# Moving VectorE's weight sums and accumulations, and two slices' splitting, inside the steps of a Strassen-like expert stage

## The reference, cut to what matters

```python
attn = top-32 attention of q, k, v               # 2 x 8 heads, 576 tokens, 64 columns
x    = ((attn @ w_a) * (attn @ w_b)) @ w_out     # 1152 tokens, 512 -> 1536 -> 512
p    = domain_probs / (domain_probs.sum(-1, keepdims=True) + 1e-9)
out  = 0
for e in range(4):                               # four experts, 512 -> 1024 -> 512
    h    = maximum(x @ w1[e], 0)
    out += p[:, e:e+1] * (h @ w2[e])
```

## Time and profile before

| | us |
|---|---|
| median of 3 runs (853.74 to 858.55) | 856.28 |
| the profiled execution, its own time | 848.76 |
| its span, first to last instruction | 847.0 |
| TensorE matmul busy in the span | 786.0 (93%) |
| VectorE busy | 578.2 (68%) |
| ScalarE busy | 432.8 (51%) |
| GpSimd busy | 362.5 (43%) |
| mean granted TensorE clock, share of full speed | 0.972 |

### The profile page before, as it was taken

How to read it: one execution, slowest core, us unless ns; L and a number is a source line. 1 busy time by engine, 2 the same in 40 slices (tenths; PEclk the granted TensorE clock), 3 DMA queues, 4 the chain that set the end, 5 groups by cost and what they waited for, 6 DMA issues and landing times. The chain is left out here.

```text
span 847.0 us, 14223 instructions
## 1 busy us (share of the span) xinstructions
PE 786.0 (93%) x5141; PEld 690.2 (81%) x5141; DVE 578.2 (68%) x1144; ACT 432.8 (51%) x848; POOL 362.5 (43%) x325
## 2 busy tenths in 40 slices
PE   4479899999999999999998799989999899989998
PEld 3357778888888888888897699789898799969987
DVE  6999998999999999995626544552456434472423
ACT  6677777777777777777545323332133323333211
POOL 2768764444444444445237102641044422363000
PEclk9668999999999999999999999999999999999999
DMA  9440684474545754445683003200032002210101
GB/s 242 123 145 27 219 286 151 145 209 163 172 152 174 232 193 158 159 156 195 226 272 105 1 26 83 68 26 1 25 100 75 1 1 75 79 47 1 51 1 62
DMA packets 80710, 97.94 MB, mean 116 GB/s; under 512 B 32896, under 2 KB 60032, under 8 KB 80640
## 3 DMA queue, kind: packets, MB, share of 16 engines
q1 hardware_dynamic: 79584, 96.77, 36.2%
q10 hardware_dynamic: 1056, 0.26, 0.1%
HBM read 86.00 MB, written 11.01 MB: 115 GB/s over the span
## 5 line engine op out<-in xcount | busy, mean ns | idle before, releaser
L730 PE MATMUL ps<-x_hi,w_hi 128*128 128x256 f32 (+1 forms) x448 | 134.6, 300 | 21.0 <-DVE u_sb L1243 15.8
L1130 DVE MAX8 m<-work 128x8 f32<-128x576 f32 x216 | 152.2, 746 | 0.0
L1263 DVE TENSOR_TENSOR c_sb<-ps,p_sb 128x256 f32<-128x256 f32 (+1 forms) x32 | 14.6, 458 | 145.8 <-PE ps L730 145.8
L798 PE MATMUL ps<-w_hi,h_hi 128*128 128x512 f32 x288 | 113.6, 394 | 0.0
L798 PE MATMUL ps<-w_lo,h_hi 128*128 128x512 f32 x288 | 113.4, 394 | 0.0
L798 PE MATMUL ps<-w_hi,h_lo 128*128 128x512 f32 x288 | 113.4, 394 | 0.0
L1364 POOL TENSOR_TENSOR p_sb<-s_sb,p_sb 128x576 f32<-128x576 f32 x72 | 101.9, 1434 | 20.4 <-ACT p_sb L876 19.8
L1136 DVE MATCH_REPLACE8 work<-m,work 128x576 f32<-128x576 f32 x144 | 105.9, 742 | 0.0
L730 PEld LDWEIGHTS ps<-x_hi,w_hi 128*128 128x128 f32 x448 | 85.3, 190 | 24.2 <-DVE u_sb L1243 17.2
L988 ACT ACTIVATE h_hi<-c_sb 128x256 fp32r<-128x256 f32 (+1 forms) x32 | 14.2, 444 | 151.6 <-DVE c_sb L1263 151.6
L1425 POOL TENSOR_TENSOR u_sb<-u_sb,p_sb 128x256 f32<-128x256 f32 (+1 forms) x32 | 31.1, 972 | 117.8 <-DVE u_sb L1256 117.8
(11 more groups left out here) (124 smaller groups left out, 2041.1 us busy)
## 6 DMA issues: line engine op xcount, KB each, us to landing
wo<-wo_d SPq DMA_DIRECT2D x96, 512.0 KB, 4.9
w_raw<-moe_w_in SPq DMA_DIRECT2D x32, 256.0 KB, 3.2
w_raw<-moe_w_in SPq DMA_DIRECT2D x16, 512.0 KB, 4.8
wo_d<-wo SPq DMA_DIRECT2D x12, 512.0 KB, 4.6
w_raw<-moe_w_a_in SPq DMA_DIRECT2D x4, 768.0 KB, 5.2
w_raw<-moe_w_b_in SPq DMA_DIRECT2D x4, 768.0 KB, 5.2
wo_raw<-moe_w_out_in SPq DMA_DIRECT2D x12, 256.0 KB, 3.4
x_d<-x_out_sb SPq DMA_DIRECT2D x9, 256.0 KB, 3.0
```

Of the source, the lines that this page charges most:

```text
L730: mm = nc.tensor.matmul(ps[:, bank, 0:NH[g]], w, x, start=first and c == n == 0, stop=last and c == HK - 1 and n == 2, skip_group_check=True)
L798: mm = nc.tensor.matmul(ps[:, DOWN_BANKS[j], 0:DM], h[:, f, tok], w[:, f, :], start=m == f == n == 0, stop=m == FM - 1 and f == 1 and n == 2)
L1130: nc.vector.max(m8[:, par, i, 8 * r:8 * r + 8], work[:, i, :]).then_inc(ve_top, 1)
```

## The change

It moves work inside the lists of three engines; no computation is added or left out, and no transfer is changed.

- `w1_prepared`: slices 2 and 3 of expert 0 are prepared in steps 1 and 2, not in steps 0 and 1. All later ones stay where they were.
- VectorE: the weight sums (and `x2_sums(1, True)` in step 2) go from the head of the step to behind the low part of h12, where TensorE has `downs(k - 1)` before it. In steps 1 and 2 VectorE also takes the low part of the raws (`w1_low_part(q, 0)`) from GpSimd. All four low pieces of x for group 1 stand in step 3, ahead of c21. The last accumulation goes behind the low parts of h22 and h21.
- ScalarE: `p5_out` goes ahead of `w2_high`; `w1_high_raws` goes from before h11 to behind h22, which itself goes ahead of both high parts; x pieces 1 to 3 go to step 3.
- GpSimd: c22 goes ahead of the low part of the raws.

```diff
         def w1_prepared(k):
             e, g, m = step(k + 2)
-            return FM * e + m if g == 0 and 2 <= k + 2 < STEPS else None
+            if 0 < k < FM - 1:
+                return k + 1
+            return FM * e + m if g == 0 and FM < k + 2 < STEPS else None
...
             def step_copies(k):
                 q1, q2 = w1_prepared(k), w2_prepared(k)
                 p1_out(k)
+                p5_out(k)
                 if q2 is not None:
                     w2_high(q2)
-                p5_out(k)
-                if q1 is not None:
-                    w1_high_raws(q1)
-                if k == FM - 2:
-                    x2_high_piece(1, 0)
-                if k == FM - 1:
-                    x2_high_piece(1, 2)
                 act.wait_ge(pe_p2, k + 1)
...
                 hidden_high(k, 0, 0, ac_h11)
                 act.wait_ge(ve_c12, k + 1)
                 hidden_high(k, 0, 1, ac_h12)
+                act.wait_ge(po_c22, k + 1)
+                hidden_high(k, 1, 1, ac_h22)
                 if q1 is not None:
+                    w1_high_raws(q1)
                     w1_high_sums(q1)
                 if k == FM - 2:
-                    x2_high_piece(1, 1)
+                    x2_high_piece(1, 0)
                 if k == FM - 1:
-                    x2_high_piece(1, 3)
-                act.wait_ge(po_c22, k + 1)
-                hidden_high(k, 1, 1, ac_h22)
+                    for i in range(1, len(X2_PIECES)):
+                        x2_high_piece(1, i)
                 act.wait_ge(ve_c21, k + 1)
                 hidden_high(k, 1, 0, ac_h21)
...
             x2_out(NT - 1)
-            w1_high_raws(2)
-            w1_high_sums(2)
             for k in range(1, STEPS):
                 step_copies(k)
...
             for k in range(STEPS):
                 done = summed_group(k - 1) if k else None
-                if k and w1_prepared(k) is not None:
-                    w1_sums(w1_prepared(k))
-                if k == FM - 2:
-                    x2_sums(1, True)
                 u2(k)
                 c12(k)
                 hidden_low(k, 0, 0, ac_h11, ve_l11)
                 u3(k)
                 hidden_low(k, 0, 1, ac_h12, ve_l12)
+                if w1_prepared(k) is not None:
+                    w1_sums(w1_prepared(k))
+                if k == FM - 2:
+                    x2_sums(1, True)
+                if 0 < k < FM - 1:
+                    w1_low_part(w1_prepared(k), 0)
                 if k == FM - 2:
                     x2_sums(1, False)
                 if k == FM - 1:
-                    x2_low_piece(1, 2)
+                    for i in range(len(X2_PIECES)):
+                        x2_low_piece(1, i)
                 if done is not None:
...
                         accumulate(e, (0, TILES[0])[g] + j)
                 c21(k)
+                hidden_low(k, 1, 1, ac_h22, ve_l22)
+                hidden_low(k, 1, 0, ac_h21, ve_l21)
                 if done is not None:
                     accumulate(e, (0, TILES[0])[g] + TILES[g] - 1)
-                hidden_low(k, 1, 1, ac_h22, ve_l22)
-                hidden_low(k, 1, 0, ac_h21, ve_l21)
-                if k == 0:
-                    w1_sums(w1_prepared(k))
-                if k == FM - 2:
-                    x2_low_piece(1, 0)
-                    x2_low_piece(1, 1)
-                if k == FM - 1:
-                    x2_low_piece(1, 3)
...
                 if q2 is not None:
                     w2_low(q2)
-                if q1 is not None and k:
-                    w1_low_part(q1, 0)
                 c22(k)
-                if q1 is not None and k == 0:
+                if q1 is not None and k >= FM:
                     w1_low_part(q1, 0)
                 if q1 is not None:
                     w1_low_part(q1, 1)
```

## The result

| | before | after |
|---|---|---|
| median of the runs | 857.16 us (4 runs, 853.74 to 858.55) | 827.0 us (4 runs, 826.24 to 827.8) |
| ratio, 95% interval | | 0.965 (0.962 to 0.969) |
| profiled execution, its own time | 848.76 | 826.24 |
| its span | 847.0 | 824.4 |
| mean granted clock in it | 0.972 | 0.979 |

Faster, by 30.2 us between the medians and by 22.5 between the profiled executions. That the two differences are not the same is the main thing to explain.

What follows compares the result with a forecast made beforehand. TensorE, busy 93% of the span, was taken as the bound, with 21.1 us of holes. Terms -6.0 - 12.7 - 1.6 = -20.3 us took the profiled 848.76 to 828.5 and the median to 836.0, range 828 to 844.

Steps and rivals of the forecast that it cites:

- What bounds the kernel: Experts' stage: TensorE, busy 93% of the span; gains only by closing holes, 21.1 us together, or keeping the clock up.
- why the six holes are there: Steps 8, 9, 16, 17, 24, 25: sums ahead of u2 stand still during GpSimd's `w2_low`; p7 waits 2.1 us each.
- Experts 1 to 3: Late steps: u2 no longer stands behind blocked sums, so the six waits of 2.1 us go; -12.7 us.
- Steps 1 to 4: Early steps of the experts' stage: p1 of step 4 comes at 481.4 instead of 487.38; -6.0 us, bounds -11.7 and 0.
- The walk by durations of single rows: Steps 1 to 3 reckoned instruction by instruction: p1 of steps 2, 3 and 4 waits 1.8, 2.0 and 1.3 us.
- the last line of the sum: Whole kernel: profiled 848.76 becomes 828.5; the median, 7.5 above the profiled execution, stays so and comes to 836.0.
- The clock term: Step 8: the low clock after its 2 us hole, one in six, goes with the hole; -1.6 us.
- Rival (b): Other executions lose more to clock drops after holes; the 7.5 us go with the holes: 828.5; chance 0.10.
- Bounds 0 and 0.8: Steps 10, 18, 26: possible wait each for u2, upper if GpSimd's two low parts leave VectorE no gap; 0 taken.
- (a): Early steps give nothing, as waits for c22, the slices and the x pieces chain up: 842; chance 0.14.
- (c): Blocked low parts make u2 of the following step late, 2 us each, six in all, giving back 12: 848; chance 0.06.
- (d): Steps 1 to 4: TensorE stays at 1.2 GHz over three holes, 31 lost, 20 gained: 867; chance 0.05.

Runs made afterwards that it cites:

- the early steps alone: Kernel before with only steps 0 to 3 and slices 2 and 3 in the new order: 848.9 us (ratio 0.995) and 845.3 us (0.993).
- the filling: Kernel with only steps 0 to 3 in the new order, plus 15 meaningless matmuls ahead of p7's wait in six late holes: 841.9 us, ratio 0.987.
- the late steps alone: Kernel before with only steps 4 to 31 in the new order, steps 0 to 3 and slices 2 and 3 unchanged: 836.1 us, ratio 0.982.
- the sums without the collision: Kernel before, but in steps 8, 9, 16, 17, 24, 25 w2's split goes to the end of ScalarE's and GpSimd's lists: 835.8 us (835.5 to 841.2).
- the low part back on GpSimd: New kernel with the low part of the raws of slices 2 and 3 returned from VectorE to GpSimd: 832.1 us, ratio 0.976.

## Why the prediction was wrong, and where it was right

**What bounds the kernel, and why the six holes are there: right.** The separation of w2's split from the sums took them away without moving the sums.

**Experts 1 to 3: right in mechanism, 1.4 us too small.** From p1 of step 4 to the last matmul the stage fell from 356.4 to 340.7 us, 15.7, where the terms were 12.7 + 1.6 = 14.3. A hole costs more than its idle time: from the last product of step 15 to the end of p7 of step 16 took 7.43 us before (638.11 to 645.54, full clock); the same seven products take 5.18 after, as in the chain above for step 8. That is 2.25 for a hole of 1.99. Step 17 gives 7.50 - 5.03 = 2.47 for 2.21. So each of the two cost 0.26 us more than its idle time, and six such make about 1.6. That this is the refilling of TensorE's pipeline is my reading; no run tests it.

**Steps 1 to 4: right.** -6.0 was reckoned, 6.4 came (487.38 - 480.58 = 6.8, of which 0.4 is that step 1 began earlier, at 443.59 instead of 443.95). The walk by durations of single rows was 0.35, 0.7 and 0.8 us late at its three places, and 0.4 of each is that it began at 444.0. Of the first two holes 1.30 us is under the 1.5 to 2.5 forecast and 1.53 at its lower end, and the wait of 0.5 us of p6 in step 3 did not come. VectorE's and GpSimd's timelines after, in steps 1 and 2:

```profile
453.01 1.22 DVE L1222 TENSOR_TENSOR w_raw_lo<-w_raw,w_hi 128x1024 fp32r<-128x1024 f32 x1 [1.13 <-ACT w_hi L951]
...
465.31 1.22 DVE L1222 TENSOR_TENSOR w_raw_lo<-w_raw,w_hi 128x1024 fp32r<-128x1024 f32 x1
466.44 2.43 DVE L1188 TENSOR_TENSOR x_raw<-x_raw 128x640 f32<-128x640 f32 x1
```

```profile
453.78 2.12 POOL L1411 TENSOR_TENSOR w_sum_lo<-w_sum,w_hi 128x768 fp32r<-128x768 f32 x1 [3.32 <-ACT w_hi L955]
...
465.70 2.49 POOL L1411 TENSOR_TENSOR w_sum_lo<-w_sum,w_hi 128x768 fp32r<-128x768 f32 x1 [3.32 <-ACT w_hi L955]
```

GpSimd's 1.85 became 2.12 and 2.49 where it began inside VectorE's 1.22, and VectorE's 0.82 became 2.43 behind it. The rule of the Trainium skill ("SBUF — State Buffer", "Who interferes with whom") that each side blocks the other holds here for the GpSimd side too. The trace before had shown only a small case: `w2_low` took 2.57 us in step 8, where it began inside a weight sum of 0.42, against 2.40 alone.

**The step that failed is the last line of the sum: "The median of the runs is 7.5 above it; with the same change it comes to 836.0".** It carried the difference between one profiled execution and the median over to the new kernel, as if it would stay. It did not: before, the median of 857.2 lay 8.4 us above the profiled execution, after, that of 827.0 lies 0.8 above it. Those 7.6 us are most of the miss of 9.9 (30.2 gained, 20.3 forecast); the other 2.2 are what the two profiles show, 1.4 from step 4 on, 0.4 in steps 1 to 3 and 0.4 ahead of step 1.

The clock term (-1.6) was sized by an execution that was itself lucky: only three of the 60 later runs of before were faster, and it had the low clock after one of its six late holes. That other executions of the same holes have it after more of them, at 1.6 us each, is shown by the two profiles of the early steps alone and by the filling. For the kernel before it is argued from there, by its times and its mean clock, as no long execution of it was traced. The new kernel has no late hole, and its eight runs lie within 1.8 us.

The rest is luck of the other sign. The median of 857.2 that the gain is counted from came out of four runs that all lay high; the 60 later ones have 850.7, against which the gain is 23 to 24 us. From 850.7 the sum of 20.3 would have come to 830.4, 3.4 too high. Whether the four were long by chance or by their chip is open.

Rival (b), at 0.10 and 828.5, comes closest, in its mechanism as far as it is shown and in its number. "Nothing in one profile speaks for it but the size" was a poor reason for so small a chance: five drops of 1.5 us was exactly what the gap between the profile and all three runs shown asked for, and the nine holes were there to hang them on.

**"Bounds 0 and 0.8" for step 10, and rivals (a), (c), (d): out.** In step 9 VectorE got its turn between GpSimd's two low parts (0.44 us at 554.45 for the low part of h22), in step 8 it was held by the second of them alone (0.99 at 543.83), so u2 was in time. After the new holes of 1.3 to 1.5 us both profiles of the new kernel show the full clock.

**`p5_out` ahead of `w2_high`, which was followed in the walk but not counted against the change:** it costs about 1 us net (827.4 against 826.3), as the order put back shows.

**Open:** why the parts do not add. Against 850.7 the late steps alone gain 14.6 and the early ones 4.6, together 19.2, where the change gains 23.3 (these are sums over three chips, whose kernels before differ by up to 1.6 us). The median of the early steps alone lies 5 us above their best run, that of the kernel before only 2 us above its best. If both are the low clock behind the same six holes, it falls more often in the kernel with the early steps changed; no run was made to take that apart. The 3 us by which the worst runs of before exceed six drops (859.8 against 848.7 + 5 x 1.6 = 856.7), and the run at 841.2 of the kernel without late holes, were not traced either.

## What to carry to other kernels

When a profiled execution is faster than every timed run, ask what it did not show before its difference is carried to the median: here idle places of TensorE of 2 us cost 2.25 in the profile and 1.6 more in some executions, each by itself. An instruction of VectorE with two SBUF inputs should not stand between GpSimd's and a product that is due; move either of the two to where TensorE has long work before it, and only as far as something else in that list is not made late. Where several parts of an operand come ready one after the other, let each product wait for the part that it reads: that, an even spread of the work and w2's split put back ahead of the copy of p5 (about 1 us of it) were together worth another 4.7 us here.

## What the runs showed of the hardware that was not expected

- The low clock after an idle place of 2.0 to 2.2 us comes and goes from one execution to the next with the same program and the same holes to 0.02 us: one drop of six in one, three of six in another, 1.6 us each. In the profiled executions it came behind 7 of 28 such places, behind all ten of 2.5 to 3.4 us (kernel before twice, the late steps alone, the sums without the collision, the low part back on GpSimd), and behind none of those of 0.5 to 1.6 us in the new kernel and the ones built on it.
- 15 useless matmuls in each such place made a kernel faster by 4.2 us in the median, since p7 came no later for them and the clock stayed up.
- A hole of 2.0 us cost 2.25, one of 2.2 cost 2.47.
